# Attention on one core: both heads of a pair per two tiles, scores in two row tiles of TensorE, Fourier corrections at full height

## What is computed

```python
# attention: B=2, H=8, S=768, head size 64; windows of 96 keys behind the query, and 8 global keys
scores = q @ k.T / 8 + bias(-slope[h] * distance), masked outside window and globals
x = softmax(scores) @ v                      # (B, S, 512) after joining the heads
# block 1: low-rank mixing along the sequence, then a feed-forward layer
u = x + (x.T @ U @ V).T;  x = u + relu(u @ w_ch1) @ w_ch2          # 512 -> 2048 -> 512
# block 2: real part of a 2-D Fourier transform, a norm, a feed-forward layer
u = x + real(fft(fft(x, axis=1), axis=2));  un = (u - mean) / sqrt(var + 1e-6)
out = u + relu(un @ w_ch1) @ w_ch2
```

## Time and profile before

| | |
|---|---|
| time before, median of 3 | 701.55 us (700.86 to 703.62) |
| profiled execution | 701.27 us, span 699.4 us |
| TensorE busy | 675.0 us, 97% |
| VectorE, ScalarE, GpSimd busy | 409.7, 329.9, 361.4 us |
| first scores of attention | 8.56 us |
| first product of round 0 | 100.64 us |
| first product of round 1 | 121.28 us |

### The profile page before, as it was taken

The page is one execution under the profiler, slowest core; times in us unless marked ns, Lnnn a source line. Parts: engine busy times, 40 slices in busy tenths (PEclk is TensorE's granted clock), DMA queues, the critical chain, the costliest instruction groups (busy, mean ns, idle before and its releaser), DMA issues.

```text
span 699.4 us, 10387 instructions
## 1 busy us (share of the span) xinstructions
PE 675.0 (97%) x3672; PEld 600.9 (86%) x3672; DVE 409.7 (59%) x930; ACT 329.9 (47%) x721; POOL 361.4 (52%) x373
## 2 busy tenths in 40 slices
PE   8999889999999999999999999999999999999998
PEld 6988789999998978887889878977888879998886
DVE  7655565555445466663687567563876664444444
ACT  4766657543333366443344475432344764344330
POOL 0411124345555799753554976454545957556611
PEclk9999989999999999999999999999999999999999
DMA  8442335101112521211211122111111122111232
GB/s 243 151 132 102 103 102 162 31 32 61 61 60 61 178 62 60 61 61 31 61 55 45 53 79 70 40 54 60 61 32 60 60 61 91 61 60 61 61 120 91
DMA packets 50532, 54.07 MB, mean 77 GB/s; under 512 B 4432, under 2 KB 37328, under 8 KB 50352
## 3 DMA queue, kind: packets, MB, share of 16 engines
q1 hardware_dynamic: 50480, 53.40, 24.1%
HBM read 53.39 MB, written 3.15 MB: 81 GB/s over the span
## 4 chain that ended last, share of the span: by engine, by line
PE 68%; ACT 10%; DVE 10%; POOL 6%; issue 4%; DVEq 0%; ACTq 0%; POOLq 0%
PE yP L758 9%; PE yP L760 8%; PE yP L759 8%; PE Yb L737 4%; PE Yb L739 4%; PE Yb L738 4%; PE aP L652 3%; PE aP L626 3%; PE Xb L737 2%; PE Xb L738 2%; PE Xb L739 2%; PE Zb L737 2%; PE Zb L738 2%; PE Zb L739 2%; ACT PB L893 2%
## 5 line engine op out<-in xcount | busy, mean ns | idle before, releaser
L519 POOL TENSOR_TENSOR WCL<-w_stage,WCH 128x512 fp32r<-128x512 f32 (+1 forms) x128 | 144.7, 1156 | 172.8 <-ACT WCH L978 172.8
L1298 DVE TENSOR_TENSOR Y<-yP,Y 128x512 f32<-128x512 f32 x192 | 129.9, 685 | 82.9 <-PE yP L760 82.1
L758 PE MATMUL yP<-WOH,hidH 128*128 128x512 f32 x384 | 153.9, 401 | 5.2 <-DVE Y L1298 5.0
L760 PE MATMUL yP<-WOH,hidL 128*128 128x512 f32 x384 | 151.5, 394 | 0.0
L759 PE MATMUL yP<-WOL,hidH 128*128 128x512 f32 x384 | 151.0, 393 | 0.0
L525 POOL TENSOR_TENSOR WOL<-o_stage,WOH 128x512 fp32r<-128x512 f32 x64 | 81.5, 1295 | 73.6 <-ACT WOH L985 73.6
L988 ACT ACTIVATE hidH<-Xb 128x384 fp32r<-128x384 f32 x64 | 31.3, 490 | 155.3 <-PE yP L760 155.2
L758 PEld LDWEIGHTS yP<-WOH,hidH 128*128 128x128 f32 x384 | 72.2, 188 | 23.9 <-DVE Y L1298 8.2
L760 PEld LDWEIGHTS yP<-WOH,hidL 128*128 128x128 f32 x384 | 72.1, 188 | 15.8
L759 PEld LDWEIGHTS yP<-WOL,hidH 128*128 128x128 f32 x384 | 72.2, 188 | 11.0
L737 PE MATMUL Yb<-UCH,WCH 128*128 128x384 f32 x192 | 65.6, 342 | 0.0
(11 more groups left out here) (218 smaller groups left out, 1302.3 us busy)
## 6 DMA issues: line engine op xcount, KB each, us to landing
w_stage<-w_in SPq DMA_DIRECT2D x128, 128.0 KB, 2.3
o_stage<-w_out SPq DMA_DIRECT2D x32, 512.0 KB, 3.3
V<-v_win SPq DMA_DIRECT2D x8, 704.0 KB, 6.6
K<-k_win SPq DMA_DIRECT2D x8, 644.0 KB, 5.3
Q<-q_t SPq DMA_DIRECT2D x16, 192.0 KB, 3.4
Y<-x_scratch SPq DMA_DIRECT2D x8, 384.0 KB
out<-Y SPq DMA_DIRECT2D x12, 256.0 KB, 3.6
CSraw<-seq_dft SPq DMA_DIRECT2D x1, 1348.0 KB, 5.5
```

What stands on the lines that cost most here:

```text
L519: nc.gpsimd.tensor_tensor(WCL[:, g % 2, u0:u1, :, :], w_stage[:, 1 + u0:1 + u1, :, :], hi32(WCH[:, g % 2, u0:u1, :, :]), ALU.subtract).the ...
L758: nc.tensor.matmul(bank[:, :], hh, WOH[:, h % 2, f, :], start=f == 0, stop=False)
L760: mm = nc.tensor.matmul(bank[:, :], hl, WOH[:, h % 2, f, :], start=False, stop=f == 1)
L1298: nc.vector.tensor_tensor(y, yP[t % 2][:, :], y, ALU.add).then_inc(s_yadd, 1)
```

## The change

Step n now treats two tiles of head n % 2 of its pair, so steps n and n+1 are both heads of the same two tiles, and a pair's three double steps go through its six tiles. Q2 holds both heads below each other without zeros, loaded with one DMA per pair. The scores of both steps are issued together at the even slot: for each tile the matmul of head 0 over rows 0 to 63, then that of head 1 over rows 64 to 127, into two banks. They wait for all reductions up to step n-1. At the odd slot TensorE issues no scores. PB and nmax get four slots for three. The norm is done per double step (24 of 256 columns instead of 16 of 384). Two banks each are used for all 36 steps before the rounds (outputs: the first 16 double steps). In the rounds, the remaining six double steps are spread over the gaps one by one: scores in a gap, transposes two and three gaps later, products with V four and five later; five gaps per double step, from gap 4 on. The later mixing starts three gaps later. In the Fourier part, high and low part lie on rows 0 and 32 of a tile that is zero elsewhere (F0S, TXS), FIX holds its constant in all rows, and one matmul over 128 rows does both.

```diff
-            Q2 = sb("Q2", [P, 2, 2, S], F32, a)
+            Q2 = sb("Q2", [P, 2, S], F32, a)
             K2 = sb("K2", [P, 2, KCOLS], F32, a)
             V2 = sb("V2", [P, 2, 2, VCHUNKS, DH], F32, a)
-            PB = sb("PB", [P, 3, 2, 2 * P], F32, a)
+            PB = sb("PB", [P, 4, 2, 2 * P], F32, a)
...
-        SB = [[aP[0], yP[0]], [aP[0]]]
-        TB = [[aP[1], yP[1]], [aP[1]]]
-        OB = [[aP[2], Zb], [aP[2]]]
+        def score_bank(n):
+            return (aP[0], yP[0])[n % 2] if n < WIDE else aP[n % 2]
+
+        def turned_bank(n):
+            return (aP[1], yP[1])[n % 2] if n < WIDE else aP[n % 2]
+
+        def value_bank(d):
+            return (aP[2], Zb)[d % 2] if d < WIDE_VALUES else aP[2]
+
...
-        for i, slot in enumerate(range(FFN_SLOT, 2 * STEPS + 3)):
-            put(1 + 2 * i, "attention", slot)
-        gap = 2 * (2 * STEPS + 3 - FFN_SLOT) + 3
+        put(1, "flip", WIDE - 2)
+        put(1, "value", WIDE - 3)
+        put(3, "flip", WIDE - 1)
+        put(3, "value", WIDE - 2)
+        put(5, "value", WIDE - 1)
+        gap = 4
+        for n in range(WIDE, 2 * STEPS, 2):
+            for late, kind, m in ((0, "score", n), (1, "score", n + 1), (2, "flip", n), (3, "flip", n + 1), (4, "value", n), (5, "value", n + 1)):
+                put(gap + late, kind, m)
+            gap += 5
+        gap += 2
...
-            first = 2 * (n % 3)
+            first = 2 * (n % 6 // 2)
...
-                for a in range(2):
-                    sp.dma_start(Q2[DH * a:DH * a + DH, n % 2, a, :], q_t[2 * n + a]).then_inc(s_pair[n % 2], 16)
+                sp.dma_start(Q2[:, n % 2, :], q_t[2 * n:2 * n + 2].rearrange("a d s -> (a d) s")).then_inc(s_pair[n % 2], 16)
...
-                sp.wait_ge(s_norm, 2 * n + 2)
+                sp.wait_ge(s_norm, 3 * n + 3)
...
+                    nc.gpsimd.memset(hi32(F0S[:, :]), 0.0).then_inc(s_csh, 1)
+                    nc.gpsimd.memset(hi32(TXS[:, :]), 0.0).then_inc(s_csh, 1)
...
+            def score(n):
+
+                if n % 2:
+                    return
+                pair = n // 6
+                if n % 6 == 0:
+                    pe.wait_ge(s_pair[pair % 2], 32 * (pair // 2 + 1))
+                if n > 0:
+                    pe.wait_ge(s_ttr, 2 * n)
+                if n >= WIDE:
+                    pe.wait_ge(*evacuated(n - 2))
+                    pe.wait_ge(*evacuated(n - 1))
+                for i, t, w in tiles(n):
+                    for h in range(2):
+                        rows = slice(DH * h, DH * h + DH)
+                        mm = nc.tensor.matmul(score_bank(n + h)[:, COLS * i:COLS * i + w], Q2[rows, pair % 2, P * t:P * t + P],
+                                              K2[rows, pair % 2, k_column(t):k_column(t) + w], start=True, stop=True)
+                        if i == 1:
+                            mm.then_inc(s_scores, 1)
+
+            def flip(n):
+
+                if n == 0:
+                    pe.wait_ge(s_ident, 16)
+                pe.wait_ge(s_exp, 2 * n + 2)
+                if 2 <= n < WIDE:
+                    pe.wait_ge(*evacuated(n - 2))
+                for x, (i, c) in enumerate(chunks(n)):
+                    mm = nc.tensor.transpose(turned_bank(n)[:, P * x:P * x + P], PB[:, n % 4, i, P * c:P * c + P], identf[:, :])
+                mm.then_inc(s_turned, 1)
+
+            def value(n):
+
+                pair, h, tile, d = n // 6, n % 2, 2 * (n % 6 // 2), n // 2
+                if n % 6 == 0:
+                    pe.wait_ge(s_pair_v[pair % 2], 16 * (pair // 2 + 1))
+                pe.wait_ge(*evacuated(n))
+                if h == 0 and d >= WIDE_VALUES:
+                    pe.wait_ge(s_norm, d)
+                elif h == 0 and d >= 2:
+                    pe.wait_ge(s_norm, d - 1)
+                for x, (i, c) in enumerate(chunks(n)):
+                    t, o = tile + i, DH * (2 * i + h)
+                    mm = nc.tensor.matmul(value_bank(d)[:, o:o + DH], PT[:, n % 2, P * x:P * x + P],
+                                          V2[:, pair % 2, h, max(2 * t - 1, 0) + c, :], start=c == 0, stop=c == 1 or t == 0)
+                mm.then_inc(s_pv, 1)
+

...
-                        nc.tensor.matmul(bank, F0H[:, cols], FIX[0:1, :], start=False, stop=False)
-                        mm = nc.tensor.matmul(bank, F0L[:, cols], FIX[0:1, :], start=False, stop=True)
+                        mm = nc.tensor.matmul(bank, F0S[:, cols], FIX[:, :], start=False, stop=True)
...
-                        nc.tensor.matmul(bank, TXH[0:1, P * i:P * i + P], ALT[0:1, :], start=False, stop=False)
-                        mm = nc.tensor.matmul(bank, TXL[0:1, P * i:P * i + P], ALT[0:1, :], start=False, stop=True)
+                        mm = nc.tensor.matmul(bank, TXS[:, P * i:P * i + P], ALT[:, :], start=False, stop=True)
...
+            def norm(d):
+
+                pair = d // 3
+                tile, c = NT * (pair // KD) + 2 * (d % 3), P * (pair % KD)
+                dve.wait_ge(s_exp, 4 * (d + 1))
+                nc.vector.tensor_scalar(pinv[:, d % 2, 0, :], psums[:, d % 4, :], 1e-9, None, ALU.add).then_inc(s_inv, 1)
+                dve.wait_ge(s_inv, 2 * d + 1)
+                nc.vector.reciprocal(pinv[:, d % 2, 1, :], pinv[:, d % 2, 0, :]).then_inc(s_inv, 1)
+                dve.wait_ge(s_inv, 2 * d + 2)
+                dve.wait_ge(s_pv, 2 * (d + 1))
+                nc.vector.tensor_tensor(Y[:, tile:tile + 2, c:c + P].rearrange("p t (h d) -> p t h d", h=2),
+                                        value_bank(d)[:, 0:4 * DH].rearrange("p (t h d) -> p t h d", t=2, h=2),
+                                        pinv[:, d % 2, 1, :].rearrange("p (t h) -> p t h", t=2).unsqueeze(3).broadcast_to([P, 2, 2, DH]), ALU.mult).then_inc(s_norm, 1)
+
...
+            def attention(slot):
+                score(slot)
+                if slot >= 2:
+                    flip(slot - 2)
+                if slot >= 5 and slot % 2 == 1:
+                    norm((slot - 5) // 2)
 
...
-    fix[0, 1:HALF:2] = 1.0
+    fix[:, 1:HALF:2] = 1.0
```

More of the change, by code:

```diff
@@ L656, in _ @@
+            def attention(slot):
+                score(slot)
+                if slot >= 2:
+                    flip(slot - 2)
+                if slot >= 3:
+                    value(slot - 3)
             last_piece = {}
@@ L804, in fourier @@
                         nc.tensor.matmul(bank, TNL[:, k, :], CDH[:, k, 0:DC], start=False, stop=False)
[L805 to L806 removed]
+                    nc.tensor.matmul(bank, TXS[:, HALF:HALF + 2], ALT[:, :], start=False, stop=True).then_inc(s_mid, 1)
                 elif what == "dim":
@@ L842, in fill @@
                 for kind, *what in FILL.get(gap, ()):
-                    if kind == "attention":
-                        attention(*what)
+                    if kind == "score":
+                        score(*what)
+                    elif kind == "flip":
+                        flip(*what)
+                    elif kind == "value":
+                        value(*what)
                     elif kind == "mix":
@@ L1204, in mixing_tables, with score @@
                 nc.vector.tensor_tensor(Vs[lo, :], Vraw[lo, :], hi32(Vs[lo, :]), ALU.subtract).then_inc(s_uvh, 1)
[L1206 to L1220 removed]
+            def score(n):
+                pair, h = n // 6, n % 2
+                dve.wait_ge(s_scores, n + 1)
+                if n % 6 < 2:
+                    dve.wait_ge(s_bias, 2 * pair + h + 1)
+                for i, t, w in tiles(n):
+                    nc.vector.tensor_tensor_reduce(out=PB[:, n % 4, i, 0:w], in0=score_bank(n)[:, COLS * i:COLS * i + w],
+                                                   in1=BT[:, pair % 2, h, min(t, 1), 0:w], scale=-(DH ** -0.5), scalar=3e38,
+                                                   op0=ALU.add, op1=ALU.min, accum_out=nmax[:, n % 4, i:i + 1]).then_inc(s_ttr, 1)
@@ L1438, in fill @@
                 for kind, *what in FILL.get(gap, ()):
-                    if kind == "attention":
-                        attention(*what)
+                    if kind == "score":
+                        score(*what)
+                    elif kind == "flip":
+                        flip(*what)
+                    elif kind == "value" and what[0] % 2 == 1:
+                        norm(what[0] // 2)
                     elif kind == "mix":
```

145 lines of the change are left out of this document (40 added, 105 removed).

## The result

The changed kernel takes 712.58 us (median of 4, 712.21 to 718.2), the kernel before 701.91 in the same comparison (700.86 to 703.62): ratio 1.0168, 95% interval 1.0114 to 1.0223. Slower by 1.7%, where 691.0 (685 to 703) was forecast. The profiled execution took 712.21 us, span 710.3. The first product of round 0 starts at 111.03 us, where the kernel before has 100.64 and about 96 was forecast.

The account below looks back on a forecast made before the run. TensorE was taken to set the pace in the attention slots and even more in the rounds; -7.3 - 4.8 - 0.2 + 2.0 = -10.3 us against 701.27 gave 691.0 us, range 685 to 703.

Parts of the forecast that it names:

- Fourier, -7.3: Fourier corrections at full height instead of one-row matmuls save array-shape switches and exposed weight loads at 14 places: -7.3 us.
- Row tiles, -4.8: Scores on two 64-row halves: each record overlaps only its predecessor, five record times instead of eight, plus two switches: -4.8 us.
- rival 3: Scores: both heads' records overlap completely, 0.77 us per full pair instead of 0.97; 688 us in all; chance 0.12.
- Waits in the 36 slots, -0.2: Slots before the rounds: waits on reductions behind first_split 9.9 us against 8.4, less 1.7 for the clock: -0.2 us.
- the low clock: Stretch from 94 to 101 us at clock 0.52 loses 3.4 us; half of that taken as gained, -1.7 us.
- The bound of +7: Upper bound of the term for waits in the 36 slots, if the waits doubled: +7 us.
- Rounds, +2.0: Attention in the rounds: transposes closer to scores, so TensorE waits 2.7 us against 0.9 before, mostly in round 0: +2.0 us.
- The bound was 5: Upper bound for attention in the rounds, if each of six pairs waits 0.8 us: +5 us.
- The start, nothing: Q2's memsets and one DMA less per pair change the start little; first reduction waits for the distance table, not K.
- 24 norms for 16, nothing: VectorE's extra norms, at most 13 us, lie in odd slots while TensorE works on the next pair: nothing; uncovered, 6 us.
- Rival 2: Overlap is there but waits give it back: low clock twice and 2 us more waits, +7, 698 us; chance 0.12.
- signs of being wrong: Score starts every 0.2 us; a clock row near 0.5 for over 7 us; or waits on reductions beyond 12 us.

Follow-up runs that it names:

- the Fourier kernel: Kernel before with only the Fourier corrections changed to one full-height matmul, attention untouched: 695.56 us, ratio 0.9915.
- the full-height forms: Score matmuls over all 128 rows: on changed kernel with splits at odd slots and norm(15) first, 701.57 us; with later flips and two Q DMAs too, 695.49 us.
- the edit of the gaps: Changed kernel with splits at odd slots and norm(15) first, plus the rounds' transposes and products with V one gap later: 695.64 us, ratio 0.9923.
- the two DMAs: Q of a pair loaded by two DMAs, one per head: on the changed kernel alone 709.46 us; on top of odd-slot splits, norm(15) first and later flips 693.42 us.
- the mended attention: Changed kernel with splits at odd slots, norm(15) first, flips and values one gap later in the rounds, Q by two DMAs: 693.42 us, ratio 0.9897.
- The experiment with pair 1: Changed kernel with SP issuing pair 1's loads behind its own read of n_local and n_global instead of ahead: 713.98 us, ratio 1.0173.
- the fill: Six unused matmuls of zeros before the first reductions' wait, on the kernel with odd-slot splits, norm(15) first, later flips, two Q DMAs: 692.99 us, ratio 0.9883.

## Why the prediction was wrong

- **Fourier, -7.3.** Right in mechanism and in size on TensorE. Measured as in the earlier trace rows at all 14 places of the Fourier kernel, the distance shrinks by 7.0 us together: 0.57 for 0.59 at the four "seq" places, 0.50 for 0.52 at the six "dim" places, 0.44 for 0.45 at the four with two columns. Of these 7.0, 5.5 arrive by landmarks and 6 by medians.
- **Row tiles, -4.8.** The assumption that a record runs only beside its predecessor was false; the overlap is complete, as rival 3 had it. The Trainium skill ("TensorE: Matmul & The Clock Gate", Measured speedup vs the span model) has about 4 ns per tile, and the starts 0.01 us apart agree. The block saves 0.70, not 0.33, and the short one 0.53 (25.12 to 25.93, against 1.34), not 0.06: 16 x 0.70 + 8 x 0.53 = 15.4 us of TensorE's time instead of 5.8. But the step from TensorE's time to the kernel's failed: the full-height forms show 2.8 to 3.5 us by landmarks, 1.3 to 2.1 by medians. That this is not far from 4.8 is luck: the saving on TensorE was put far too low, and the part of it that arrives far too high.
- **Waits in the 36 slots, -0.2.** This is the step that failed most. The mechanism and all seven places were named: waits of 1.1, 0.1, 1.1, 0.1, 1.8, 1.8 and 1.8 us were forecast behind the splits of slots 14, 16, 20, 22, 26, 28 and 32, 7.8 together. They measured 1.90, 0.42, 1.90, 0.42, 2.62, 1.86 and 2.62, 11.7 together, and moving the splits by one slot made round 0 come 11.2 us earlier. Two errors made it small. The first is the price: the chain of VectorE and ScalarE was sized nearly right (from the scores of slot 14 at 42.62 to those of slot 16 at 47.85 are 5.2 us, 5.0 were forecast), but TensorE's own work in between was put at 3.9 and is 3.3, because the block takes 0.98 and not 1.35. A gain on TensorE turns into wait at once. The second is the low clock, booked as a gain of 1.7 where one stretch was to shorten: it came in seven. The bound of +7, "waits doubled", was nearer.
- **Rounds, +2.0.** Mechanism right (ScalarE at the first flip of the rounds: forecast 1.6, measured 2.0), size too small: the edit of the gaps alone gives back 3.9 by landmarks, 4.6 by medians. The bound was 5.
- **The start, nothing.** That one DMA less per pair changes the start little was false and was never costed: 3.7 us at the first cast, 3.1 (medians) to 3.9 (landmarks) at the end. The first reduction does wait for the distance table and not for K, as stated; what was left out is that the table waits for a register load, and that this load takes longer when the transfers are issued in the other form and order.
- **24 norms for 16, nothing.** Nearly: TensorE waits 3.2 once at the norm before the rounds, but moving that norm gains 0.4 to 0.6 by landmarks and nothing by medians.
- **Sum.** At round 6 the changed kernel stands 15.8 us behind the Fourier kernel. From the one profile to the next, splits and norm take 11.1 off, the gaps of the flips 3.9, the two DMAs 1.0 (3.6 where nothing else is mended), and 2.7 are two executions' difference ahead of round 0. That makes 18.7; the 2.9 over 15.8 are what the mended attention gains, if it gains anything. Rival 2 (the waits give the overlap back, with low clock) was the mechanism, at 0.12 and with a third of its size: the time came 21.6 above the forecast, not 7. Two of the signs of being wrong came: the clock at its lower level for over 7 us (13.7 at the start), and waits on the reductions beyond 12 us (14.7).

What stays open: how much of the 16.4 is clock and how much is wait. The experiment with pair 1 shows a stretch at 1.2 GHz that costs time, since TensorE is busy all through it; the fill moved such a stretch without removing it; those of the changed kernel weren't separated from the waits ahead of them. Open too is what slows the register load.

## What to carry to other kernels

Time taken from an engine counts only up to the next engine of the same slot. Work out first whose chain then ends last, since here 10 us saved on TensorE in the slots came to about 1 us at round 0. When a wait is widened to "all work of the last step", move whatever stands in that engine's queue ahead of that work to the slot that does not feed the wait: one slot was worth 11 us. When the first transfers of a kernel change, look in the trace at the small loads that every engine waits for: here one DMA less made them end 3.7 us later. And before a landmark of two kernels is compared, look whether both executions started alike.

## What the runs showed of the hardware

- Two f32 matmuls on different 64-row halves overlap completely, both records of each and their weight loads: starts at most 0.01 us apart, the pairs 0.19 to 0.30 us behind each other, eight records in 0.98 us.
- Leaving the tiled shape costs an exposed load: 0.29 us idle of the load unit at 29.62.
- The first part of an engine's register load from DRAM took 1.1 us in three kernels with two DMAs for Q and 2.4 in a fourth with the same issue times, and 3.7 to 3.8 us in seven with one. SP's own took 0.50 us with 361 GB/s moving.
- TensorE's clock at 1.2 GHz can last while it is busy without a break: 24 to 41 us in the pair 1 experiment.
